# Routing counts of a mixture-of-experts kernel as rounded products, and the last expert's second tile one step further behind

## What is computed

```
expert_idx = np.argmax(logits, axis=1)
for i in range(N):
    e = expert_idx[i]
    if counts[e] < capacity:
        disp[e, counts[e]] = x[i]
        pos[i] = counts[e]
        counts[e] += 1
        keep[i] = True
h = np.maximum(np.einsum('ecd,edf->ecf', disp, w1), 0.0)
y = np.einsum('ecf,efd->ecd', h, w2)
for i in range(N):
    if keep[i]:
        out[i] = gate_w[i] * y[expert_idx[i], pos[i]]
```

## Time and profile before

| what | value |
|---|---|
| time, median of 3 runs | 423.93 us (423.81 to 423.94) |
| profiled execution | 423.77 us, span 422.0 us |
| TensorE (PE) busy | 411.6 us, 98% |
| TensorE's weight loads (PEld) busy | 394.2 us, 93% |
| VectorE (DVE) busy | 243.0 us, 58% |
| ScalarE (ACT) busy | 187.6 us, 44% |
| GpSimd (POOL) busy | 233.0 us, 55% |

### The profile page before, as it was taken

One profiled execution on the slowest core, in us unless ns is written; L12 is line 12 of the kernel. 1 busy time (PEld: TensorE's weight loads), 2 busy tenths in 40 slices (PEclk: granted clock), 3 DMA queues, 4 the chain that ended last, 5 costly groups with the idle time before them and its releaser, 6 DMA issues.

```text
span 422.0 us, 9143 instructions
## 1 busy us (share of the span) xinstructions
PE 411.6 (98%) x3553; PEld 394.2 (93%) x3553; DVE 243.0 (58%) x576; ACT 187.6 (44%) x407; POOL 233.0 (55%) x241
## 2 busy tenths in 40 slices
PE   8898999999999999999999999999999999999994
PEld 8798799999999999999999998998999999999994
DVE  7888654484576456645653477686536455364521
ACT  4776453323333332333333455553556455564520
POOL 3788766638657855685562325146082652826531
PEclk9999999999999999999999999999999999999998
DMA  7999978304030403020008001735463935639000
GB/s 250 402 396 417 373 218 288 114 2 153 2 116 16 141 2 116 7 99 2 0 23 333 4 0 39 256 139 181 185 254 119 360 117 241 256 113 357 7 32 28
DMA packets 18649, 64.97 MB, mean 154 GB/s; under 512 B 2203, under 2 KB 11717, under 8 KB 16432
## 3 DMA queue, kind: packets, MB, share of 16 engines
q1 hardware_dynamic: 16816, 59.68, 38.8%
q0 software_dynamic: 1792, 4.73, 3.0%
HBM read 51.98 MB, written 13.21 MB: 154 GB/s over the span
## 4 chain that ended last, share of the span: by engine, by line
PE 81%; DVE 6%; issue 4%; POOL 4%; ACT 2%; DMA 1%; SPq 0%; POOLq 0%
PE bank L1343 24%; PE bank L1345 22%; PE bank L1344 22%; PE bank L1361 2%; DVE wd_lo L1041 1%; POOL g_lo L694 1%; DMA rkt<-rkt 1%; DVE elu L1171 1%; PE bank L1425 1%; PE bank L1429 1%; PE bank L1389 1%; ACT elu L847 1%; PE bank L1662 1%; PE bank L1418 1%; DVE elu L1163 1%
## 5 line engine op out<-in xcount | busy, mean ns | idle before, releaser
L694 POOL TENSOR_TENSOR g_lo<-elu,g_hi 128x256 fp32r<-128x256 f32 x95 | 72.3, 761 | 94.8 <-ACT g_hi L854 94.2
L1343 PE MATMUL bank<-xt,wd_hi 128*128 128x256 f32 x285 | 80.8, 284 | 1.9 <-DVE elu L1171 1.9
L1345 PE MATMUL bank<-xt,wd_lo 128*128 128x256 f32 x285 | 80.3, 282 | 0.0
L1344 PE MATMUL bank<-xt,wd_hi 128*128 128x256 f32 x285 | 80.3, 282 | 0.0
L847 ACT ACTIVATE elu<-elu 128x256 f32<-128x256 f32 x96 | 40.1, 418 | 90.3 <-DVE elu L1163 89.8
L1171 DVE SCALAR_TENSOR_TENSOR elu<-elu,bank 128x256 f32<-128x256 f32 x96 | 40.3, 420 | 50.4 <-ACT elu L847 49.6
L1343 PE MATMUL bank<-wd_hi,g_hi 128*128 128x392 f32 (+1 forms) x192 | 68.3, 356 | 0.3 <-ACT x2row L815 0.3
L1345 PE MATMUL bank<-wd_hi,g_lo 128*128 128x392 f32 (+1 forms) x192 | 65.1, 339 | 0.0
L1344 PE MATMUL bank<-wd_lo,g_hi 128*128 128x392 f32 (+1 forms) x192 | 65.1, 339 | 0.0
L1163 DVE TENSOR_SCALAR elu<-bank 128x256 f32<-128x256 f32 x80 | 33.7, 422 | 42.6 <-PE bank L1345 41.8
L854 ACT CAST g_hi<-elu 128x256 fp32r<-128x256 f32 x96 | 38.9, 406 | 43.4 <-DVE elu L1171 43.3
(11 more groups left out here) (218 smaller groups left out, 954.4 us busy)
## 6 DMA issues: line engine op xcount, KB each, us to landing
we_raw<-wexp SPq DMA_DIRECT2D x8, 1536.0 KB, 6.9
wd_raw<-wexp SPq DMA_DIRECT2D x8, 1536.0 KB, 7.3
rkt<-rkt SPq DMA_DIRECT2D x12, 512.0 KB, 5.3
nat<-nat SPq DMA_DIRECT2D x9, 672.0 KB, 4.0
xrow<-slots SPq DMA_DIRECT2D x16, 193.0 KB, 7.2
wd_raw<-win SPq DMA_DIRECT2D x4, 768.0 KB, 9.2
wd_raw<-wout SPq DMA_DIRECT2D x4, 768.0 KB, 9.8
wo_tr<-wouttr SPq DMA_DIRECT2D x1, 3072.0 KB, 17.3
```

Source lines behind the costliest of these rows:

```text
L694: nc.gpsimd.tensor_tensor(g_lo[:, f % 4, :], elu[:, f % 2, :], g_hi[:, f % 4, :].bitcast(F32), ALU.subtract).then_inc(s_glo, 1)
L1343: mm(dst, w_hi, x_hi, start=start, stop=False)
L1344: mm(dst, w_hi, x_lo, start=False, stop=False)
L1345: return mm(dst, w_lo, x_hi, start=False, stop=stop)
```

## The change

Two edits. The first makes the three kinds of count products from rounded operands: ScalarE casts `ones` and `earlier` to fp32r once at the start, VectorE writes the one-hot, `before` and `n_seen` as fp32r (whole numbers, which it can hold), and every count waits for the casts too (`s_round`). The two new tiles take 1 KB per partition, for which a scratch tile (`wg_tr`) is laid over the tile that has been read when it is written (`wo_tr`). The second edit puts tile 1's second-layer products of the last expert one step further back.

```diff
+    earlier_r = new("earlier_r", [128, 128], F32R)
+    ones_r = new("ones_r", [128, 128], F32R)
...
-    onehot = new("onehot", [128, BT, NE])
-    before = new("before", [128, BT, NE])
-    n_seen = new("n_seen", [128, NE])
+    onehot_r = new("onehot", [128, BT, NE], F32R)
+    onehot = onehot_r[:, :, :].bitcast(F32)
+    before_r = new("before", [128, BT, NE], F32R)
+    before = before_r[:, :, :].bitcast(F32)
+    n_seen_r = new("n_seen", [128, NE], F32R)
+    n_seen = n_seen_r[:, :].bitcast(F32)
...
-    wo_tr, wg_at = put("wo_tr", [128, KT, DFF], F32, wo_at)
-    wg_tr, end_g = put("wg_tr", [128, GCOL], F32, wg_at)
+    wo_tr, end_g = put("wo_tr", [128, KT, DFF], F32, wo_at)
+    wg_tr = put("wg_tr", [128, GCOL], F32, wo_at)[0]
...
+        s_round = sem("count_operands_ready")
...
+            act.wait_ge(s_const, NPOOLC)
+            nc.scalar.copy(ones_r[:, :], ones[:, :]).then_inc(s_round, 1)
+            nc.scalar.copy(earlier_r[:, :], earlier[:, :]).then_inc(s_round, 1)
             act.wait_ge(s_tables, NTAB)
...
-                link(V.tensor_copy(before[:, 0, :], n_seen[:, :]))
+                link(V.tensor_copy(before_r[:, 0, :], n_seen[:, :]))
...
-                link(V.tensor_tensor(onehot[:, :, :], key[:, :, :], bc(col3[:, 0, :].unsqueeze(2), full), ALU.is_equal))
-                V.tensor_tensor(before[:, 1, :], before[:, 0, :], onehot[:, 0, :], ALU.add).then_inc(s_oh, 1)
+                link(V.tensor_tensor(onehot_r[:, :, :], key[:, :, :], bc(col3[:, 0, :].unsqueeze(2), full), ALU.is_equal))
+                V.tensor_tensor(before_r[:, 1, :], before[:, 0, :], onehot[:, 0, :], ALU.add).then_inc(s_oh, 1)
                 dve.wait_ge(s_oh, n + 1)
-                V.tensor_tensor(n_seen[:, :], before[:, 1, :], onehot[:, 1, :], ALU.add).then_inc(s_seen, 1)
+                V.tensor_tensor(n_seen_r[:, :], before[:, 1, :], onehot[:, 1, :], ALU.add).then_inc(s_seen, 1)
...
             def count(n):
 
+                pe.wait_ge(s_round, 2)
                 pe.wait_ge(s_oh, n + 1)
                 wait_if(pe, s_row, n)
                 pe.wait_ge(s_xlo, 2 * min(2 * n + 5, NSTEP))
                 if n in (EB - 1, NB - 1):
                     pe.wait_ge(s_seen, n + 1)
-                    mm(ps_tot, ones[:, :], n_seen[:, :], start=True, stop=True)
-                mm(ps_cnt, earlier[:, :], onehot[:, :, :], start=True, stop=False)
-                mm(ps_cnt, ones[:, :], before[:, :, :], start=False, stop=True).then_inc(s_pos, 1)
+                    mm(ps_tot, ones_r[:, :], n_seen_r[:, :], start=True, stop=True)
+                mm(ps_cnt, earlier_r[:, :], onehot_r[:, :, :], start=True, stop=False)
+                mm(ps_cnt, ones_r[:, :], before_r[:, :, :], start=False, stop=True).then_inc(s_pos, 1)
...
-                    if f >= 2:
+                    if more and f >= 2:
                         fc2_expert(i, r, f - 2)
+                    if not more:
+                        for t in range(2):
+                            if f >= 2 + t:
+                                fc2_expert(i, r, f - 2 - t, (t,))
...
                 else:
                     for t in range(2):
-                        fc2_expert(i, r, ET - 2, (t,))
-                        fc2_expert(i, r, ET - 1, (t,))
+                        for f in range(ET - 2 - t, ET):
+                            fc2_expert(i, r, f, (t,))
```

## The result

The changed kernel takes 422.28 us (median of 6 runs, 421.92 to 422.56) against 423.91 us (6 runs, 423.62 to 423.94): a ratio of 0.9964 (95% interval 0.9953 to 0.9975, from here on written in brackets), 1.63 us less by the medians. The forecast was 422.4 us. The profiled execution took 422.56 us, its span 420.7 us, 1.3 us less than the span before.

A forecast was written before the change was run, and what follows sets the result against it. The prediction took TensorE, busy for 98% of the span, as the bound. Counts 1.30 us plus the end of the kernel 0.23 us made 1.53 us, so 423.93 - 1.53 = 422.4 us, own range 421.9 to 422.9.

The forecast's parts named there:

- 14 passes less, 0.112 us each: In the six counts, each rounded product runs one pass instead of two, taking 1.57 us off TensorE's queue.
- half a load: Rival: a rounded count product costs only 0.056 us, half a plain weight load; 421.9 us in all, chance 0.06.
- two passes: Rival: narrow rounded products still run twice through TensorE, so rounding gives 0; 423.7 us, chance 0.13.
- Count 1, 0.18 us: At the count near 86.6 us, 0.22 us is saved, but VectorE's idle time lets only 0.18 us through.
- Count 2: At the count near 124.4 us, TensorE waits for no other engine behind it, so all 0.22 us arrives.
- Counts 3 and 4, 0.34 and 0.22 us: Three products at the count near 166.6 us and two at the next; both savings were taken whole.
- Count 5, nothing: TensorE comes 0.22 us earlier but waits 0.22 us longer for VectorE, which also splits the first expert's weights.
- Count 6: At the count near 274.3 us, three products save 0.34 us whole; the picks are ready 0.08 us before TensorE wants them.
- The new wait at 0: Waiting for the one-hot ahead of each count product costs 0; 0.26 us was kept for the range.
- The slower rival: Rival: TensorE's instruction stream, held at each of the six counts, runs dry; 425.1 us at 0.45 us a count, chance 0.07.
- The tail, 0.23 us: After the last product, tile 0 ends 0.52 us earlier, but tile 1's scaling and scatter limit the gain to 0.23 us.
- The rival that other engines swallow it: Rival: VectorE and GpSimd hold the pace behind counts 1 to 4, leaving 0.57 us; 423.4 us, chance 0.12.

## Why the prediction was right, and where it was off

- **14 passes less, 0.112 us each: right.** 14 records fewer, load starts 0.11 us apart, and eight narrow products in 0.89 us. The rivals of half a load and of two passes fall with the same rows. The Trainium skill, "FP8 and Floating Point Precision", section "TensorE Precision Notes", gives true FP32 four passes; the trace has two records for a plain product and the cost of two loads. "TensorE: Matmul & The Clock Gate", in the section on weight-path perf modes, gives a load of 128 weights about twice the speed where the type isn't FP32; the rounded loads here start 0.11 us apart, as the plain ones do.
- **Count 1, 0.18 us: right in kind, 0.15 measured.** VectorE's step came 0.15 us earlier and no more: 0.03 of the 0.18 us stand between its instructions anyway.
- **Count 2, "TensorE stands still for no other engine up to the next count; taken whole": wrong.** 0.05 us came of 0.22. The step that failed is reading the absence of a stall as freedom to move. GpSimd's `nat` was finished at the very moment when TensorE's loads ahead of it were, and it hangs on the routing's chain, not on TensorE: the wait for it took 0.13 of the 0.17 us. The reading itself was not quite right either. Behind count 2 the kernel before has one idle time that the view puts down to another engine:

```profile
137.13 0.19 PEld L1343 LDWEIGHTS bank<-wd_hi,g_hi 128*128 128x128 f32 x1 [0.20 <-POOL g_lo L694]
```

That one took nothing: the changed kernel has it too, 0.20 us long at 136.77, and its advance is 0.07 us ahead of it and behind it.
- **Counts 3 and 4, 0.34 and 0.22 us: right,** 0.33 and 0.19.
- **Count 5, nothing: right,** by the idle time of 0.44 for 0.22 us, by the plain count there, and by three more products, which left the distance to count 6 as it was.
- **Count 6, "whole, with 0.08 us to spare": 0.30 of 0.34.** The picks are ready in time, and their load waits for nothing; 0.03 us are missing right behind the count, and why is open. The 0.08 us to spare were counted to the record of TensorE's product (276.67), whose load had started 0.11 us before it; that the load still waits for nothing is luck, since it stands only 0.12 us behind the picks' last write.
- **The new wait at 0: right.** Distances with it and without it agree within 0.04 us, count by count. The slower rival, a stream that runs dry, falls.
- **Casts at 0: right,** hidden with 2.45 us left.
- **The tail, 0.23 us: 0.30 measured.** That tile 1's own path takes over as the bound is right, and so is tile 0's gain (0.51 for 0.52 us). The mis-sized term is the 0.86 us from scaling to scatter: tile 1 needs 0.80, so the scatters are 1.50 us apart and not 1.57. What makes the difference of 0.06 is not shown.
- **The rival that other engines swallow it** came true at one of the four counts that it named, count 2.
- **The sum** forecast 1.53 us. By the traces it is 1.02 + 0.30 = 1.32; the two profiled executions differ by 1.21 us, and the medians by 1.63 with an interval from 1.06 to 1.99 (0.25% to 0.47% of 423.91). That 422.28 lies so near 422.4 owes something to the spread of the runs: the traces' sum would put it at 422.6.

## What to carry to other kernels

Price a narrow matmul by the start distance of weight loads: halving the passes of a float32 product saved one load of 0.11 us for each product of 8 or 16 columns, and a rounded product of 128 columns cost no more than one of 16. For each stretch that gets shorter, don't ask only whether the bounding engine waits in it; ask of each operand behind it when it was finished, and on whose pace it hangs. An operand that was ready just in time swallows the gain without having shown a stall. With savings of some tenths of a microsecond, compare distances between fixed marks in many traces; the span moves more than that by itself.

## What the runs showed of the hardware

- A scatter on GpSimd started 0.86 us behind the end of the scaling when GpSimd had been idle for over 11 us, and 0.80 us when its previous scatter had ended 0.53 us before (in three kernels or more each); where the tile had long been ready, the second scatter followed the first with 0.30 us between.
- ScalarE scales a 128x384 tile from PSUM in 0.58 us, VectorE in 0.62: moving such a step to the idle ScalarE bought 0.03 us.
- Sixteen loads of the outer products, set between the dense layer's loads instead of directly behind the attention's, cost 0.2 us more: their first load starts 0.33 us behind the layer's last, where layer loads follow each other by 0.12.
- A wait that stands alone ahead of a product held TensorE's instruction stream for up to 2.1 us at a count, while the loads ahead of it in the queue went on. At count 2 it ended 0.14 us before the count's load, which started 0.12 us behind the one before. The record of these waits in the changed kernel (six; ns min/median/max, first and last start):

```profile
L1561 PEldq EVENT_SEMAPHORE  x6: 51/778/2103, 85.5 to 269.5; - x6
```
